# One-core linear attention and two channel mixers: loads spaced out, level masks as a bitwise and, decay products on GpSimd

## The chip, the cores and the metric

The kernel runs on one core of a Trainium2 chip. The metric is device time in microseconds of one execution; the kernel before took 908.53 us (median of three runs, 905.54 to 910.15).

## The reference, cut to what matters

Four batches, eight heads, 768 tokens, head width 48, everything float32. Three stages follow each other:

```
state = alpha[t] * state + outer(k[t], v[t]);  y[t] = q[t] @ state        # linear attention, per head
x = y, heads side by side (384 wide)
xk, xr = token-shifted mixes of x;  k = relu(xk @ w_k);  x = sigmoid(xr @ w_r) * (k*k @ w_v)
u = x + token mixing of x through U, V (rank 32);  out = u + relu(u @ w_ch1) @ w_ch2
```

## The kernel before, in words

**Units.** One unit of attention is half a batch: 384 tokens of 8 heads, n = 2b + half, eight units in all. Q and K lie feature by token in `QK` with two groups g = 0, 1 of 768 columns, and alpha in `T`. The causal attention inside a chunk of 128 tokens is built up over levels of doubling blocks: TensorE multiplies K and Q blocks (`in_half`, L419, 96 small matmuls a level), VectorE copies the wanted blocks of the result into `Pm` under a byte mask (`keep`, L1029), then multiplies Q and K by the decay products (L1060 for level step 0, L1065 for the others) and doubles the decay products themselves (`double_T`, L1035). `keep` has three forms, by the block width B: B = 1 (levels 0 and 1), B = 2 (level 2, with the two inner axes exchanged), B of 4 and more (levels 3 to 5). Levels 6 and 7 are copied by ScalarE (L787, L791). `Pm` starts as zeros (L1243; the second unit has its own `Pm_2`, L1296), so that masked places stay zero. After the levels TensorE turns K (L475), multiplies `Pm` by v (L483), forms the change of state per chunk (L510), VectorE carries the states along (`end_states`, L1082 and L1095), and TensorE adds what comes from the state (L526).

**Weights in two parts.** Every product of the mixers is three fp32r matmuls, high x high, low x high, high x low (L594 to L596). So each weight is split once: ScalarE makes the high part (L928), and a subtraction makes the low part: on VectorE for six of the pieces of w_k and w_v (L1239), on GpSimd for w_r, one piece each of w_k and w_v, and all twelve pieces of w_ch1 and w_ch2 (L1302).

**Order of the work.** Each engine's program is written out by hand. Unit 0 runs alone. After that, attention of the next unit is cut into 13 steps (a generator), and the plans `FIRST`, `BESIDE1`, `BESIDE_T`, `BESIDE2`, `BESIDE3` say how many steps come ahead of each slice f of the mixers, on all engines alike. `channel_mix` is the first mixer (8 slices f, with hidden squares made by VectorE at L1170 and L1173), `mlp` the second (12 slices, L1215). `mix` prepares their inputs (ACT L862, DVE L1148, L1143). Half (0, 0) is straight code, with attention of unit 1 beside it. A hardware loop over b = 0 to 2 then does `channel_mix(b,1)`, `token_mix(b)`, `mlp(b,0)` beside attention of unit (b+1, 0), and `channel_mix(b+1,0)`, `mlp(b,1)` beside unit (b+1, 1). The rest of batch 3 follows with no attention beside it. TensorE meets the steps of `keep`, L1065 and the hidden squares through semaphores; VectorE does them in one queue, in program order.

**The start.** SyncE issues the loads of q, k and alpha of unit 0, then at once all of mu, w_r, w_k, v, V, the six tensors of unit 1, w_v, U and w_ch1 (L339 to L378). w_ch2 is loaded at L355 after unit 1 is done, as its raw copy lies over `Pm_2`. In `attend_first` the first attention step of unit 1 (`next(other)`, its diagonal) stands on TensorE ahead of the turning of K and on VectorE ahead of `end_states` of unit 0. ScalarE makes the high parts of w_v partly after unit 0 (`run(highs)`).

Of the kernel before, what the change touches and what calls it, by code (L numbers as in the profile page):

```python
# [31 lines left out]
U8 = mybir.dt.uint8  # L32
ALU = mybir.AluOpType
# [7 lines left out]
def build(nc, q, k, v, alpha, mu_in, w_k, w_v, w_r, U, V, w_ch1, w_ch2, out):  # L41
# [21 lines left out]
    with ctx:  # L63
# [16 lines left out]
        with ExitStack() as first:  # L80
            def early(name, shape):
                return first.enter_context(nc.sbuf_tensor(name, shape, F32))

            QK_2 = early("QK_2", [P, 2, 2 * S])
            T_2 = early("T_2", [P, 2 * S])
            raw = [early(f"raw_{name}", [P, *shape]) for name, shape in (
                ("k", (KT, F1 * P)), ("r", (KT, DM)), ("v", (F1, DM)), ("1", (KT, F2 * P)))]
            with nc.sbuf_tensor("Pm_2", [P, 2 * NC, 2, P], F32) as Pm_2:
                pass
            raw.append(early("raw_2", [P, F2, DM]))  # L90
            masks = early("masks", [P, 2, MW])
# [11 lines left out]
        level_mask = sb("level_mask", [P, MW], U8)  # L103

# [20 lines left out]
        class Unit:  # L125
            QK: object
            T: object
            Pm: object
# [18 lines left out]
        def states(qk, at):  # L147
# [3 lines left out]
            Unit(QK, T, Pm, [vt[:], by_chunk(x1_flat[:, HC * DM:HC * DM + NC * HP])], [states(QK, 0), states(QK, 1)]),  # L151
            Unit(QK_2, T_2, Pm_2, [vt[:], by_chunk(QK_2[:, 1, 0:NC * HP])], [states(QK_2, 0)] * 2),
            Unit(QK, T, Pm, [vt[:], by_chunk(QK[:, 1, 0:NC * HP])], [states(QK, 0)] * 2),
# [33 lines left out]
        s_zero, s_zero_2 = sem("zero"), sem("zero_2")  # L187
# [4 lines left out]
        s_wld = [sem(f"w{i}_loaded") for i in range(5)]  # L192
# [7 lines left out]
        s_second = pair("second_loaded")  # L200
# [3 lines left out]
        s_qk, s_T = pair("QK_doubled"), sem("T_doubled")  # L204
# [96 lines left out]
        def loaded(eng, n, s, g):  # L301

            if isinstance(n, int) and n == 1:
                eng.wait_ge(s_second[g], 48)
# [11 lines left out]
        def _(sp):  # L316
# [35 lines left out]
            def load_w(i, src, parts):  # L352
                n = src.shape[1]
                for j in range(0, n, n // parts):
                    sp.dma_start(raw[i][:, j:j + n // parts, :], src[:, j:j + n // parts, :]).then_inc(s_wld[i], 16)  # L355
# [12 lines left out]
            load_w(1, w_r, 1)  # L368
            load_w(0, w_k, 3)
            load_v(0, 0, 0)  # L370
            load_v(0, 0, 1)
            sp.dma_start(V_raw, V).then_inc(s_V, 16)
            for g in range(2):
                sp.dma_start(part(units[1].K(), g), k[0, 1, g]).then_inc(s_second[g], 16)
                sp.dma_start(part(units[1].Q(), g), q[0, 1, g]).then_inc(s_second[g], 16)
                sp.dma_start(part(T_2[0:HR], g), alpha[0, 1, g]).then_inc(s_second[g], 16)
            load_w(2, w_v, 2)
            sp.dma_start(u_sb[:], U).then_inc(s_U, 16)  # L378
            load_w(3, w_ch1, 3)
# [34 lines left out]
        def _(pe):  # L414
# [63 lines left out]
            def own(n, g, h, c, z, q0, q1):  # L478

                u = unit(n)  # L480
                for e in range(2):
                    cc, keys = h * HC + c, slice(z * HS, (z + 1) * HS)
                    mm = pe.matmul(y_bank(n, g, h)[e * HS:e * HS + D, c * P + q0:c * P + q1], u.vt[g][keys, cc, e, :],  # L483
                                   u.Pm[keys, g * NC + cc, e, q0 - z * HS:q1 - z * HS],
# [74 lines left out]
            def attend_first(steps, other):  # L559
# [4 lines left out]
                next(other)  # L564
# [25 lines left out]
                from_state(n, half, 1)  # L590

# [125 lines left out]
            def mlp(b, half, step, plan, acc_free, turns=()):  # L717
                s = 2 * b + half
                for f in range(F2):
                    step(plan[f])  # L720
                    if f == 0 and half == 0:
                        pe.wait_ge(s_plo, NR + 2 + 2 * N1)
# [52 lines left out]
        def _(act):  # L775
            def levels(n):
                Pm = unit(n).Pm
# [23 lines left out]
            def attention(b, half):  # L801
# [3 lines left out]
                act.wait_ge(s_T, LV * (n + 1))  # L805
                for g in range(2):
                    for h in range(2):
# [16 lines left out]
            def attend_first(steps, highs):  # L824


                for _ in range(ML + 2):
                    next(steps)
                    next(highs, None)
                next(steps)  # L830
                next(highs)
# [98 lines left out]
            def early_weights():  # L930

                act.wait_ge(s_wld[1], 16)
                for n in range(NR):
                    high(n, *PIECES[n][:2])
                yield
# [3 lines left out]
                yield  # L939
                act.wait_ge(s_wld[0], 48)  # L940
                for n in range(NR, NR + NK):
                    high(n, *PIECES[n][:2])
                    if n % 2 == 0:
                        yield
                yield
                yield
                yield
                act.wait_ge(s_wld[2], 32)
                for n in range(NR + NK, NR + 2 * NK):
                    high(n, *PIECES[n][:2])  # L950
                    if n == NR + NK:
                        yield

            def later_weights():

                act.wait_ge(s_wld[3], 48)
# [4 lines left out]
            def last_weights():  # L961

                act.wait_ge(s_y[1], 4)
                act.wait_ge(s_split, 64 * KT)
                act.wait_ge(s_wld[4], 48)
                for n in range(NE + N1, NE + 2 * N1):
                    high(n, *PIECES[n][:2])
# [3 lines left out]
            highs = early_weights()  # L971
            attend_first(levels(0), highs)
            steps = together(attention(0, 1), later_weights(), [1] * 13, N1)
            step = stepper(steps)
            step(START)
            run(highs)
# [26 lines left out]
        def _(dve):  # L1003
# [399 lines left out]
```

## Time and profile before

| | |
|---|---|
| profiled execution, own time | 905.27 us |
| its span, first to last instruction | 903.5 us |
| TensorE busy | 801.7 us (89%) |
| VectorE busy | 475.6 us (53%) |
| ScalarE / GpSimd busy | 272.5 / 39.4 us |
| mean granted TensorE clock | 0.941 of full |

A busy share says how much of the span an engine had an instruction under way. TensorE is near full over most of the span; the holes lie in the first 176 us and once in each half of the loop.

### The profile page before, as it was taken

To read this page: it belongs to the slowest core of one execution; us is meant where nothing else is said; L and a number is where in the kernel's file an instruction comes from. 1 tells how busy PE (TensorE), PEld (TensorE's weight loads), DVE (VectorE), ACT (ScalarE), POOL (GpSimd) and SP (SyncE) were. 2 spreads that over 40 slices of the span, in tenths; PEclk is the share of its full clock that TensorE was granted. 3 is DMA by queue.
4 is the path that set the end of the run, shared out by engine and by line. 5 is a ranking of instruction groups with operands and counts; after the bars stand their busy time and mean duration, and the time that the engine had idled before them with its cause. 6 is when DMAs were issued, how large, how long until landed. Compare 5 with 4: busy or idle time off the path is not lost.

```text
span 903.5 us, 24726 instructions
## 1 busy us (share of the span) xinstructions
PE 801.7 (89%) x10680; PEld 744.0 (82%) x10680; DVE 475.6 (53%) x797; ACT 272.5 (30%) x555; POOL 39.4 (4%) x40
## 2 busy tenths in 40 slices
PE   4656985798998998798998999889999899998998
PEld 4556875687998898796997989787899889997998
DVE  6668837864277624765247732676328651533132
ACT  1234334234241413223232333213333142421121
POOL 2040028000000000000000000000000000000000
PEclk9977896899999999889999999889999999999999
DMA  9600024000400012000120004000120000000000
GB/s 273 219 21 3 2 90 141 2 2 16 111 28 3 15 52 89 2 2 15 52 89 1 3 18 108 29 2 1 50 77 28 1 15 8 27 1 1 1 27 26
DMA packets 15602, 37.32 MB, mean 41 GB/s; under 512 B 2544, under 2 KB 6512, under 8 KB 15504
## 3 DMA queue, kind: packets, MB, share of 16 engines
q1 hardware_dynamic: 15408, 35.72, 13.2%
q8 instruction: 88, 1.44, 0.7%
q10 hardware_dynamic: 96, 0.07, 0.0%
q14 instruction: 10, 0.08, 0.0%
HBM read 29.89 MB, written 4.72 MB: 38 GB/s over the span
## 4 chain that ended last, share of the span: by engine, by line
PE 76%; DVE 16%; issue 5%; ACT 2%; DMA 1%; DVEq 0%; SPq 0%; ACTq 0%
PE acc L594 11%; PE acc L595 10%; PE acc L596 10%; PE hps L594 9%; PE hps L595 8%; PE hps L596 8%; PE aps L419 7%; DVE Pm L1029 4%; DVE QK L1065 4%; PE aps L483 2%; PE aps L526 2%; PE hps L682 2%; DVE T L1035 1%; PE aps L475 1%; DVE QK L1060 1%
## 5 line engine op out<-in xcount | busy, mean ns | idle before, releaser
L1215 DVE SCALAR_TENSOR_TENSOR hid_l<-hps,hid_h 128x384 fp32r<-128x384 f32 x96 | 53.5, 557 | 215.6 <-ACT hid_h L922 215.6
L1065 DVE TENSOR_TENSOR QK<-QK,T 112x768 f32<-112x768 f32 x96 | 92.2, 974 | 42.2 <-PE aps L419 36.7
L419 PEld LDWEIGHTS aps<-QK 48*64 48x64 f32 x4704 | 82.4, 146 | 37.1 <-issue 37.1
L922 ACT ACTIVATE hid_h<-hps 128x384 fp32r<-128x384 f32 x96 | 47.2, 492 | 207.9 <-PE hps L596 207.9
L419 PE MATMUL aps<-QK 48*64 48x32 f32 x4704 | 88.1, 230 | 23.5 <-DVE Pm L1029 9.9
L594 PE MATMUL hps<-in_h,w_h 128*128 128x384 f32 x288 | 100.2, 348 | 1.0 <-DVE in_l L1191 0.9
L596 PE MATMUL hps<-in_h,w_l 128*128 128x384 f32 x288 | 96.9, 337 | 0.0
L595 PE MATMUL hps<-in_l,w_h 128*128 128x384 f32 x288 | 96.9, 336 | 0.0
L596 PE MATMUL acc<-w_h,hid_l 128*128 128x384 f32 x288 | 96.4, 335 | 0.0
L594 PE MATMUL acc<-w_h,hid_h 128*128 128x384 f32 x288 | 96.3, 334 | 0.0
L595 PE MATMUL acc<-w_l,hid_h 128*128 128x384 f32 x288 | 96.2, 334 | 0.0
L888 ACT ACTIVATE tmp<-hps 128x384 f32<-128x384 f32 x64 | 31.5, 492 | 187.1 <-PE hps L596 156.8
L594 PE MATMUL acc<-wv_h,hid_h 128*128 128x384 f32 x192 | 68.9, 359 | 21.1 <-DVE hid_l L1173 21.1
L1029 DVE COPY_PREDICATED Pm<-level_mask,aps 128x384 f32<-128x384 uint8 x84 | 78.7, 937 | 0.0
L594 PE MATMUL hps<-in_h,wk_h 128*128 128x384 f32 x192 | 72.1, 376 | 3.4 <-DVE in_l L1143 3.4
L595 PE MATMUL acc<-wv_l,hid_h 128*128 128x384 f32 x192 | 67.1, 349 | 0.0
L596 PE MATMUL acc<-wv_h,hid_l 128*128 128x384 f32 x192 | 67.0, 349 | 0.0
L596 PE MATMUL hps<-in_h,wk_l 128*128 128x384 f32 x192 | 66.9, 348 | 0.0
L595 PE MATMUL hps<-in_l,wk_h 128*128 128x384 f32 x192 | 66.9, 348 | 0.0
L594 PEld LDWEIGHTS acc<-wv_h,hid_h 128*128 128x128 f32 x192 | 38.1, 199 | 26.8 <-DVE hid_l L1173 23.6
L1170 DVE TENSOR_TENSOR hid_h<-tmp 128x384 fp32r<-128x384 f32 x64 | 37.0, 578 | 41.8 <-ACT tmp L888 41.8
L594 PEld LDWEIGHTS hps<-in_h,w_h 128*128 128x128 f32 x288 | 54.6, 190 | 4.9 <-issue 2.2
(147 smaller groups left out, 1365.9 us busy)
## 6 DMA issues: line engine op xcount, KB each, us to landing
QK<-in_k SPq DMA_DIRECT2D x16, 336.0 KB, 4.2
QK<-in_q SPq DMA_DIRECT2D x16, 336.0 KB, 5.4
T<-in_alpha SPq DMA_DIRECT2D x16, 336.0 KB, 5.7
raw<-in_w_ch SPq DMA_DIRECT2D x6, 768.0 KB, 13.5
out<-x SPq DMA_DIRECT2D x24, 192.0 KB, 1.9
vt<-in_v SPq DMA_DIRECT2D x8, 288.0 KB, 4.3
QK<-in_v SPq DMA_DIRECT2D x7, 288.0 KB, 2.8
raw_k<-in_w_k SPq DMA_DIRECT2D x3, 512.0 KB, 9.8
```

Of the source, the lines that this page charges most:

```text
L419: return pe.matmul(to[z * HS:(z + 1) * HS, at:at + W2], u.K()[rows, cols], queries(u.Q()[rows, cols]), start=True, stop=True)
L483: mm = pe.matmul(y_bank(n, g, h)[e * HS:e * HS + D, c * P + q0:c * P + q1], u.vt[g][keys, cc, e, :], u.Pm[keys, g * NC + cc, e, q0 - z * H ...
L526: mm = pe.matmul(y_bank(n, g, h)[rows, c * P:(c + 1) * P], before, u.Q()[rows, t0:t0 + P], start=False, stop=(c == HC - 1))
L594: pe.matmul(o, a[0], b[0], start=first, stop=False)
L595: pe.matmul(o, a[0], b[1], start=False, stop=False)
L596: return pe.matmul(o, a[1], b[0], start=False, stop=last)
L888: nc.scalar.activation(tmp[:, 0, :], hps[f % 2][:, 0:HT], ACT.Relu).then_inc(s_rel, 1)
L922: nc.scalar.activation(hid[0][:, f % 2, :], hps[f % 2][:, 0:HT], ACT.Relu).then_inc(s_rel2, 1)
L1029: nc.vector.copy_predicated(to, m, src).then_inc(s_keep, 1)
L1065: nc.vector.tensor_tensor(qk, qk, t, ALU.mult).then_inc(s_qk[g], 1)
L1170: nc.vector.tensor_tensor(hid[0][:, f % 2, :], tmp[:, 0, :], tmp[:, 0, :], ALU.mult).then_inc(s_hh, 1)
L1215: nc.vector.scalar_tensor_tensor(out=hid[1][:, f % 2, :], in0=hps[f % 2][:, 0:HT], scalar=0.0, in1=hid[0][:, f % 2, :].bitcast(F32), op0=A ...
```

## The change

- **Loads**: nearly every load after the first six waits for the landing of the one two before it, so that two are under way; w_ch2 is loaded after w_ch1, not after unit 1. Semaphores are per part.
- **Masks**: `whole_mask` holds 0 or -1 as int32 (two small GpSimd instructions). For levels 0 and 1 `keep` writes all places with `bitwise_and` of the PSUM result and this mask, from PSUM to `Pm`. Levels 2 to 5 keep `copy_predicated`; the exchanged form for B = 2 is gone, so level 2 uses the form of levels 3 to 5. The clearing of `Pm` and all of `Pm_2` are gone; all units share `Pm`.
- **Decay products**: `double_T` leaves VectorE. GpSimd has a stream `attention(n)` for each unit, with the same products per group g (14 instructions a unit), waiting for `s_Ke[g]` or `s_qk[g]`, with a loop of its own over b.
- **Unit 1's diagonal**: `next(other)` moves behind unit 0's `from_state(…,1)` on TensorE and behind `end_states` and the copies of y on VectorE.
- **Low parts**: the twelve pieces of w_ch1 and w_ch2 go from GpSimd to VectorE: six in the steps beside half (0, 0) (`LOWS`), six after it (`last_lows`).
- **High parts**: ScalarE makes w_r, w_k and V ahead of unit 0's level copies and w_v between these and the copies of y; w_ch1 follows `HIGHS`. The high parts of w_ch2 stay after `mix(0,1,0)`.
- **Plan**: `FIRST` brings unit 1's steps forward: [0,1,2,1,2,1,2,1,2,0] becomes [0,1,2,2,2,2,2,1,0,0].

```
-                if B == 1:
-                    to, src = to[:, :, :, 0], src[:, :, :, 0]
-                    m = m.unsqueeze(1).to_broadcast([P, 2 * NC, k])
-                elif B == 2:
-                    to, src = (x.rearrange("p c n b -> p c b n") for x in (to, src))
-                    m = m.unsqueeze(1).unsqueeze(1).to_broadcast([P, 2 * NC, B, k])
-                else:
-                    m = m.unsqueeze(2).unsqueeze(1).to_broadcast([P, 2 * NC, k, B])
+                if lev < 2:
+                    m = whole_mask[:, mask_at(lev):mask_at(lev) + k].unsqueeze(1).to_broadcast([P, 2 * NC, k])
+                    nc.vector.tensor_tensor(to[:, :, :, 0].bitcast(I32), src[:, :, :, 0].bitcast(I32), m,
+                                            ALU.bitwise_and).then_inc(s_keep, 1)
+                    return
+                m = m.unsqueeze(2).unsqueeze(1).to_broadcast([P, 2 * NC, k, B])
                 nc.vector.copy_predicated(to, m, src).then_inc(s_keep, 1)
...
+            def attention(n):                                    # GpSimd
+                t = unit(n).T[0:HR]
+                for l in range(LV):
+                    B = 1 << l
+                    for g in range(2):
+                        part_t = part(t, g)
+                        t_left, t_right = part_t[:, B - 1:S:2 * B], part_t[:, 2 * B - 1:S:2 * B]
+                        if l == 0:
+                            pool.wait_ge(s_Ke[g], n + 1)
+                        else:
+                            pool.wait_ge(s_qk[g], LV * n + l + 1)
+                        to = t_right
+                        if l == LV - 1:
+                            to = T_end[:, g * NC:(g + 1) * NC]
+                            ge(pool, s_st[g], 4 * n)
+                        nc.gpsimd.tensor_tensor(to, t_right, t_left, ALU.mult).then_inc(s_T[g], 1)
+                    yield
...
-            load_w(1, w_r, 1)
-            load_w(0, w_k, 3)
+            sp.wait_ge(s_ldq[1], 16)
+            load_part(rw, w_r, 0, KT, s_wr)
+            sp.wait_ge(s_lda[1], 16)
+            load_part(kw, w_k, 0, 1, s_wk[0])
+            sp.wait_ge(s_wr, 16)
+            load_part(kw, w_k, 1, 1, s_wk[1])
...
             sp.wait_ge(s_y[0], 2)
             load_v(0, 1, 0)
+            for i in range(3):
+                sp.wait_ge(s_w1[i], 16)
+                load_part(w2w, w_ch2, i * F2 // 3, F2 // 3, s_w2[i])
             load_v(0, 1, 1)
             move_split(0, 1)
-            sp.wait_ge(s_y[1], 4)
-            load_w(4, w_ch2, 3)
...
             run(steps)                                           # VectorE, after channel_mix(0, 0)
+            last_lows()
```

## Rows read from the trace of the kernel before

**Rows 1.** Windows by part of the program: start:end, length, busy us, clock, DMA

```profile
0.00:66.00 66.00, 38.62 (x1028) 35.08 (x1028) 41.93 (x61) 15.52 (x27) 15.69 (x28) 0.91 0.57 176
66.00:133.00 67.00, 55.64 (x993) 51.48 (x994) 43.93 (x72) 29.26 (x58) 2.79 (x2) 0.83 0.06 16
133.00:176.00 43.00, 25.99 (x367) 23.83 (x366) 36.14 (x37) 14.45 (x27) 20.90 (x11) 0.76 0.31 100
176.00:783.00 607.00, 567.83 (x7665) 525.16 (x7665) 318.36 (x563) 186.89 (x391) 0.00 (x0) 0.96 0.11 31
```

**Rows 2.** TensorE in order of time; in brackets the idle before, and its releaser

```profile
279.98 0.69 PE L594 MATMUL acc<-wv_h,hid_h 128*128 128x384 f32 x1 [3.06 <-DVE hid_l L1173]
...
359.98 1.32 PE L419 MATMUL aps<-QK 48*64 48x32 f32 x75 [2.21 <-issue]
...
374.29 1.68 PE L419 MATMUL aps<-QK 48*64 48x32 f32 x96 [0.39 <-DVE Pm L1029]
383.91 0.44 PE L594 MATMUL acc<-wv_h,hid_h 128*128 128x384 f32 x1 [3.06 <-DVE hid_l L1173]
```

**Rows 3.** Windows around two of these waits

```profile
276.00:286.00 10.00, 6.94 (x119) 6.23 (x118) 6.05 (x9) 1.01 (x2) 0.00 (x0) 0.83 0.00 0
380.00:394.00 14.00, 10.94 (x156) 9.87 (x157) 9.18 (x14) 2.04 (x4) 0.00 (x0) 0.76 0.01 1
```

**Rows 4.** VectorE in order of time, ahead of the wait at 276.9

```profile
264.47 1.01 DVE L1029 COPY_PREDICATED Pm<-level_mask,aps 128x384 f32<-128x384 uint8 x1
...
276.36 1.84 DVE L1029 COPY_PREDICATED Pm<-level_mask,aps 128x384 f32<-128x384 uint8 x1
277.81 1.07 DVE L1035 TENSOR_TENSOR T<-T 112x384 f32<-112x384 f32 x1
...
285.76 0.57 DVE L1029 COPY_PREDICATED Pm<-level_mask,aps 128x384 f32<-128x384 uint8 x1
```

**Rows 5.** Groups of instructions: busy, mean ns, idle before

```profile
L1035 DVE TENSOR_TENSOR T<-T 112x768 f32<-112x768 f32 x8 | 8.7, 1092 | 0.0
L1184 DVE TENSOR_TENSOR x<-acc,x 128x384 f32<-128x384 f32 x24 | 12.3, 553 | 9.4 <-PE acc L596 9.4
```

**Rows 6.** One line on VectorE: duration in ns, least, median, most

```profile
L1045 DVE TENSOR_TENSOR QK<-QK,T x16: 553/558/2205, 7.5 to 685.4; 112x384 f32<-112x384 f32 x16
```

**Rows 7.** The chain that ended last, 22 to 66 us: start, length, what

```profile
22.75 2.94 issue
...
30.04 2.56 issue
...
37.29 1.56 issue
...
65.04 2.29 ACT wv_h L928 x3
```

**Rows 8.** GpSimd and VectorE beside each other, 48 to 57 us

```profile
51.79 2.12 POOL L1302 TENSOR_TENSOR wv_l<-raw_v,wv_h 128x768 fp32r<-128x768 f32 x1
...
52.16 1.01 DVE L1029 COPY_PREDICATED Pm<-level_mask,aps 128x384 f32<-128x384 uint8 x1
52.98 1.75 DVE L1035 TENSOR_TENSOR T<-T 112x768 f32<-112x768 f32 x1
```

**Rows 9.** TensorE and VectorE in order of time, 56 to 163 us

```profile
56.89 1.09 PE L526 MATMUL hps<-QK 48*48 48x128 f32 x8 [4.21 <-DVE carry L1095]
...
132.40 1.87 DVE L1170 TENSOR_TENSOR hid_h<-tmp 128x384 fp32r<-128x384 f32 x1 [4.10 <-ACT tmp L888]
...
153.10 4.28 DVE L1045 TENSOR_TENSOR QK<-QK,T 112x384 f32<-112x384 f32 x2
...
144.75 1.51 PE L419 MATMUL aps<-QK 48*64 48x32 f32 x48 [5.10 <-DMA QK<-in_k]
...
162.89 0.69 PE L594 MATMUL hps<-in_h,wk_h 128*128 128x384 f32 x1 [2.84 <-DVE in_l L1143]
```

**Rows 10.** DMA issues: kind, count, KB each, us to landing

```profile
QK<-in_k SPq DMA_DIRECT2D x16, 336.0 KB, 4.2
```

More of the change, by code:

```diff
@@ L32 @@
 U8 = mybir.dt.uint8
+I32 = mybir.dt.int32
 ALU = mybir.AluOpType
@@ L199, in build @@
         s_ldq, s_ldk, s_lda, s_ldv = (pair(f"{n}_loaded") for n in "qkav")
[L200 removed]
+        s_q2, s_k2, s_a2 = (pair(f"second_{n}_loaded") for n in "qka")
         s_dg, s_Ke = pair("even_diagonal"), pair("K_even_ready")
@@ L350, in move_split, with load_part @@
                                      unit(n).y_split()[e * HS + 16 * i:e * HS + 16 * (i + 1), :]).then_inc(s_split, 16)
[L352 to L355, printed above, removed]
+            def load_part(raw_w, src, i, n, done):
+                sp.dma_start(raw_w[:, i:i + n, :], src[:, i:i + n, :]).then_inc(done, 16)
             def store(b, half):
@@ L367, in _ @@
             sp.dma_start(mu[:, 0:2, :], mu_in).then_inc(s_mu, 16)
-            load_w(1, w_r, 1)
-            load_w(0, w_k, 3)
+            sp.wait_ge(s_ldq[1], 16)
[4 more added lines that the diff above has]
+            load_part(kw, w_k, 1, 1, s_wk[1])
+            sp.wait_ge(s_wk[0], 16)
+            load_part(kw, w_k, 2, 1, s_wk[2])
+            sp.dma_start(V_raw, V).then_inc(s_V, 16)
+            sp.wait_ge(s_wk[1], 16)
             load_v(0, 0, 0)
+            sp.wait_ge(s_wk[2], 16)
             load_v(0, 0, 1)
[L372 to L377, printed above, removed]
-            sp.dma_start(u_sb[:], U).then_inc(s_U, 16)
-            load_w(3, w_ch1, 3)
+            sp.wait_ge(s_ldv[0], 16)
+            load_part(vw, w_v, 0, F1 // 2, s_wv[0])
+            sp.wait_ge(s_ldv[1], 16)
+            load_part(vw, w_v, F1 // 2, F1 // 2, s_wv[1])
+            Q2, K2 = units[1].Q(), units[1].K()
+            sp.wait_ge(s_wv[0], 16)
+            sp.dma_start(part(K2, 0), k[0, 1, 0]).then_inc(s_k2[0], 16)
+            sp.wait_ge(s_wv[1], 16)
+            sp.dma_start(part(Q2, 0), q[0, 1, 0]).then_inc(s_q2[0], 16)
+            sp.wait_ge(s_k2[0], 16)
+            sp.dma_start(part(K2, 1), k[0, 1, 1]).then_inc(s_k2[1], 16)
+            sp.wait_ge(s_q2[0], 16)
+            sp.dma_start(part(Q2, 1), q[0, 1, 1]).then_inc(s_q2[1], 16)
+            sp.wait_ge(s_k2[1], 16)
+            sp.dma_start(part(T_2[0:HR], 0), alpha[0, 1, 0]).then_inc(s_a2[0], 16)
+            sp.wait_ge(s_q2[1], 16)
+            sp.dma_start(part(T_2[0:HR], 1), alpha[0, 1, 1]).then_inc(s_a2[1], 16)
+            sp.dma_start(u_sb[:], U).then_inc(s_U, 16)
+            sp.wait_ge(s_a2[0], 16)
+            load_part(w1w, w_ch1, 0, 1, s_w1[0])
+            sp.wait_ge(s_a2[1], 16)
+            load_part(w1w, w_ch1, 1, 1, s_w1[1])
+            sp.wait_ge(s_w1[0], 16)
+            load_part(w1w, w_ch1, 2, 1, s_w1[2])
             move_split(0, 0)
@@ L590, in attend_first @@
                 from_state(n, half, 1)
+                next(other)
             def three(o, a, b, first, last):
@@ L822, in attention, with attend_first @@
                     yield
[L824 to L831, printed above, removed]
+            def attend_first(steps):
+                first_weights()
+                run(steps)
+                next_weights()
                 for g in range(2):
@@ L1045, in levels @@
                     nc.vector.tensor_tensor(k_even, k_even, t_odd, ALU.mult).then_inc(s_Ke[g], 1)
-                keep(n, 0, 0)
-                dve.wait_ge(s_Ke[1], n + 1)
-                double_T(n, 0)
-                keep(n, 0, 1)
+                for e in range(2):
+                    keep(n, 0, e)
                 yield
@@ L1122, in attend_first @@
                         ).then_inc(s_kt[g], 1)
-                dve.wait_ge(s_zero_2, 1)
-                next(other)
                 end_states(0, 0, 0)
@@ L1132, in attend_first @@
                         nc.vector.tensor_copy(to, y_bank(0, g, h)[rows, 0:HT]).then_inc(s_xe, 1)
+                next(other)
             def mix(b, half, what, between=lambda: None):
@@ L1302, in low @@
                 nc.gpsimd.tensor_tensor(w_lo, src, w_hi.bitcast(F32), ALU.subtract).then_inc(s_plo, 1)
-            pool.wait_ge(s_qk[1], LV)
+            run(attention(0))
             for n in (*range(NR + 1), NR + NK):
@@ L1312, in _ @@
             pool.wait_ge(s_vst, 3)
-            pool.wait_ge(s_y[1], 4)
-            for n in range(NE, NE + 2 * N1):
-                low(n, n)
-FIRST = [0, 1, 2, 1, 2, 1, 2, 1, 2, 0]
+            run(attention(1))
+            with pool.Fori(1, NB) as b:
+                run(attention(2 * b))
+                run(attention(2 * b + 1))
+FIRST = [0, 1, 2, 2, 2, 2, 2, 1, 0, 0]
 BESIDE1 = [1, 1, 1, 0, 1, 1, 0, 1, 1, 0]
```

121 lines of the change are left out of this document (55 added, 66 removed).

## The prediction

> **What bounds the kernel now.** I read the windows by part of the program first, since a mean over the span hides where time is lost. From 176 to 783 us TensorE is busy 567.8 of 607 us at clock 0.96, [rows 1]; the 120.5 us after it have no attention and are not touched. Ahead of that it is idle 27.4, 11.4 and 17.0 us in three parts that end at 176 us, at clocks of 0.91, 0.83 and 0.76. So there are two places: the opening, and whatever opens the 39 us of holes in the loop. TensorE's own order of time shows these: one wait of 3.06 us in each half with attention beside it, always for the hidden square's low part on VectorE [rows 2]; it occurs five times after 176 us, at 280, 384, 492, 596 and 703. Behind each the granted clock falls to 1.2 GHz for a while: the stretch reads 0.83 over 10 us in three cases, 0.76 over 14 us in two [rows 3], which is 1.7 and 3.4 us of work lost each, 11.9 in all. VectorE's rows show why it is late: from 262 (or 372) on it runs with no gap, and hid_h and hid_l stand in its queue behind two level-2 keeps of 1.8 us and a T of 1.07 us [rows 4]. VectorE at 53% busy is thus the bound for some 18 us of every half.
>
> **Masks.** A keep of level 0 or 1 takes 1.01 us and one of level 2 1.84, one of level 3 0.57, for the same 384 elements [rows 4]; starts of neighbours are 0.92, 1.78 and 0.47 us apart, as neighbours overlap by about 0.1. The bitwise and is a two-operand instruction with 384 elements. The nearest rows are the PSUM add, 0.553 us [rows 5], and the product with a step of two elements, 0.558 us [rows 6]: 0.47 net. Upper bound: no gain, 0.92. I take 0.47, since both output step and source are as in these rows. Saved: 0.45 each, four a unit. Level 2 in the plain form writes pairs of elements; the level-0 form writes every second element, also two in each four, so I put it at 0.93, with bounds 0.47 (level 3) and 1.78 (no gain). Saved: 0.85 each, two a unit.
> The Trainium skill, "SBUF — State Buffer", section on port mapping, says two hits in a 16-byte line suffice for full bandwidth; by that rule level 2 would cost 0.47 too. The level-0 keep has two hits in a line and takes twice a level-3 keep, so for this instruction the row speaks against the rule; by the rule about 0.4 us more would be saved a keep, most of it where no wait is left.
>
> **T on GpSimd.** VectorE loses T: 0.99 at step 0 (eight in 8.7 us, one of them stretched to 1.75 [rows 5, 8]), 1.07 at step 1 [rows 4], then 0.5, 0.33, 0.24, 0.2, 0.18. On GpSimd a two-operand subtraction of 768 columns takes 2.12 us [rows 8], 2.75 ns a column; T of one group has 384, 192, 96, ... products, so 1.06, 0.53, 0.26 us and little after: 4.1 us a unit. Bounds: as on VectorE below, three times as much above, since no row has GpSimd with a step. It is needed one step later, over 3 us on, so it hides. What it touches is VectorE: while GpSimd ran its 2.12 us, VectorE's T, with two SBUF inputs, took 1.75 in place of 1.0, whereas the keep beside it, with PSUM as source, took its usual 1.01 [rows 8]. So only products and in_l/hid operations can be held up, for at most one GpSimd instruction. By the queue order T(0,g) runs beside the two ands and touches in_l by up to 1 us, T(1,g) and later ones run beside the keep that follows their product: nothing. I take 0.3 us a unit.
> The Trainium skill, "SBUF — State Buffer", section on who interferes with whom, says that a DVE instruction with two SBUF inputs and a GpSimd one that reads SBUF exclude each other fully. The rows above agree for the two-input case, and with the exemption of one-input ones. Taken as a rule against this change, all GpSimd time could land on VectorE; that is the first rival.
>
> **The loop, five halves.** In the three halves of the 280 kind VectorE's full run starts before step 0 (262), and loses 0.9 + 0.99 + 0.9 + 1.7 + 1.07 = 5.5 us ahead of hid_l, more than the 3.06 wait. In the two of the 384 kind the run starts at 372, and loses 0.9 + 1.7 + 1.07 = 3.7, against 3.06 plus 0.39 that TensorE itself comes earlier, its wait for the level-1 keep being gone [rows 2]; after handoffs I leave 0.3. Sum: 3 x 3.06 + 2 x 3.15 = 15.5. Of the 11.9 lost by the clock I take 9, as other gaps (2.21 us, instruction supply, at the loop's end [rows 2], and one before u is turned) stay. Small ones: 0.5. Together 25. If an edit brings less than its share, the wait comes back with the clock.
>
> **Opening, unit 0 (to 47).** VectorE's run up to 22 us loses 0.9 + 0.8 + 0.9 + 1.7, of which TensorE's two matmul halves of 1.5 us a step leave 3. Behind it stand three gaps of TensorE in which nothing but instruction supply is late, 2.94 + 2.56 + 1.56 = 7.1 [rows 7], while the loads fill the DMA engines (they end with them). Spaced loads bring between nothing and all of it, or lose if loads come late: 16 landings up to the first part of w_ch1, two under way, 4.2 us each [rows 10], end at about 10 + 16 x 2.1 = 44 us, ahead of the move of y behind it in SP's queue (58 before, about 50 after); w_r, w_k, w_v land by 30 and are wanted at 40 or later. With a third more each it would be 55, and the move about 5 us late. I take 1.5, so 4.5 for this part.
> **47 to 68.** The diagonal's work on VectorE (48.78 to 55.4, stretched by GpSimd [rows 8]) leaves the path from K's turning to the states. What is late next is TensorE: turning the states of group 1 ends at 52.7, so its 4.21 us gap before the state product [rows 9] goes and some of the 1.2 GHz time after it: 6. High parts of w_v and one of w_ch1 behind the last y, 2.29 [rows 7] + 0.82, go: 3.1. Given back: products and ands of the diagonal ahead of mix, 4 x 0.47 = 1.9. Together 7.
> **68 to 139.5.** The run of VectorE from 78.3 to 102.8 loses 0.9 + 1.7 + 2.3 (T of steps 1 to 4) = 4.9. The plan that brings steps forward changes only order: VectorE has 27 us of work to the end of step 6, TensorE 18 us. At 133 TensorE waits 3.0 us for hid_l while GpSimd's subtractions stretch hid_h to 1.87 [rows 9] and runs at 1.2 GHz for 3 us: 4.5 back, as no subtraction is left there. Six w_ch1 subtractions at 0.87 move to VectorE where it is 60 to 70% idle: 1 lost (0 to 5). Together 8.4.
> **139.5 to 162.89.** This is 23.4 us for TensorE, with a 5.1 us wait for K behind w_ch2 and two-input operations of 2 us each on VectorE [rows 9]. After, K is there, and the chain is VectorE's: mix 2.6, three products 1.5, six w_ch2 subtractions 5.2, two sums of mix 1.1, products and ands 1.9, in_l 0.5, ACT and sum 1.2, in_l twice 1.1, handoffs 0.2: 15.3. Saved 8.1. The wait of 2.5 at 173 goes as in the loop: 2.5. Without that chain's subtractions it would be 13; beside GpSimd nothing now.
>
> **Sum.** 4.5 + 7 + 8.4 + 8.1 + 2.5 + 25 = 55.5. Own time 905.3 - 55.5 = 849.8; the median of the runs is 3.3 above the profiled one, so 853.
>
> **Rivals.**
> 1. *The port takes it back.* GpSimd's T of steps 0 and 1 is 3.2 us a unit; if each holds up a two-input operation in VectorE's full run, eight units lose 25 us: about 879. For: rows 8 and 9. Against: the queue order puts keeps, which aren't held up, beside nearly all of them.
> 2. *The masks cost as before.* If the and takes 0.92 and level 2 1.78, only T leaves the run: the loop's waits shrink by 3 x 2.06 + 2 x 1.07 = 8.3 and the clock gives 4, so 12.3 in place of 25; the opening loses about 3.5: 869. For: no row has an int32 operation or the pair form. Against: same element counts as in rows 5.
> 3. *Slower.* GpSimd's product with a step costs three times the contiguous one, 8 ns an element: T is 12.3 us a unit, T(0,g) 3.1 each. They then stand before the step-0 products and hold up mix: the run grows by 9.3 - 5.5 = 3.8 in each of 6 halves, with the clock 23 to 30 on top of the present time, and about 10 in units 0 and 1, against 28 kept in the opening: about 915. It turns at some 8 ns an element. For: the step is new. Against: the row shows 2.75.
> 4. *The start stays as it is.* If instruction supply and late loads bind TensorE up to the first mix as before, 4.5 + 7 go: 865. For: the gaps end with the loads. Against: the 4.21 us gap waits for VectorE, not for a load [rows 9].
>
> **Chances.** Forecast 0.64, first 0.13, second 0.10, fourth 0.07, slower 0.04; 0.02 for no change. Between 0.5% either way this kernel can't be told from itself. Range: rivals 1, 2 and 4 reach to 879; below, all supply gaps, the whole clock and no port loss are 5.6 + 2.9 + 2.4 + 3 = 14, so to 839; rounding errors of the hand count widen it: 834 to 882. The forecast's own range is 838 to 865. Faster 0.93, same 0.02, slower 0.05.
>
> **What would show it.** On TensorE's order of time no wait over 0.5 us for L1173 in the loop; clock near 1 where it read 0.83; level-2 keeps near 0.93 and ands near 0.56; T on GpSimd near 1.06 and 0.53, and no L1143 or L1065 above 1.2 us beside it; mix of half (0,0) begins by 57; f = 0 of half (0,1) about 30 us earlier, near 133. Wrong: hid_l waits that stay with the old length, in which case the run of VectorE was not what I took it for, or TensorE waiting for SP's move of y.

## The result and the profile after

The changed kernel takes 854.24 us (median; 851.68 to 855.22), against 909.29 of the kernel before: ratio 0.940, 95% interval [0.936, 0.943]. The forecast of 853 with "faster" was right. The profiled execution took 855.14 us with a span of 853.4, and between the two profiled executions the gain is 50.1 us where the prediction added up 55.5: the opening gave 24.4 us instead of 30.5, the loop 26 instead of 25. That the median still came within 1.3 us of the forecast is luck, see below.

One line of TensorE separates the two well: the 24 matmuls with `v_stack` in the low-rank product of the MLP, the first behind the opening, the last near the end. Before and after (count; least, median and longest duration in ns; first and last start in us):

```profile
L700 PE MATMUL acc<-hid_h,v_stack x24: 334/414/689, 207.0 to 822.3; 96*128 96x384 f32 x24
```

```profile
L723 PE MATMUL acc<-hid_h,v_stack x24: 334/416/686, 182.6 to 771.9; 96*128 96x384 f32 x24
```

Below, the first number is called the opening (207.0 to 182.6) and the difference the loop (615.3 to 589.3). In the ten kernels below that leave the loop as the change made it, it is 589.1 to 590.0, so it repeats from profile to profile within 1 us. The opening does not: unit 0's y is ready at 43 us in e5, e7 and e8 and at 47 after the change, though the code up to there is the same.

Windows by part of the program, as in [rows 1] (start:end, length, busy us of TensorE, its weight loads, VectorE, ScalarE and GpSimd, then clock, DMA share and GB/s):

```profile
0.00:58.00 58.00, 37.25 (x1031) 33.86 (x1031) 31.67 (x57) 18.78 (x33) 21.18 (x45) 0.95 0.77 240
58.00:121.00 63.00, 54.98 (x991) 50.44 (x991) 42.80 (x69) 25.86 (x52) 6.44 (x12) 0.88 0.17 47
121.00:149.00 28.00, 21.23 (x348) 19.97 (x349) 23.16 (x38) 13.55 (x25) 2.95 (x4) 0.76 0.01 3
149.00:733.00 584.00, 561.30 (x7686) 519.51 (x7685) 291.11 (x526) 188.66 (x395) 41.05 (x80) 0.98 0.12 33
```

In the loop TensorE is busy 96% at clock 0.98, where it was 94% at 0.96. The three parts of the opening are shorter, and still at 0.95, 0.88 and 0.76.

TensorE's order of time, where [rows 2] had 3.06 us, and the window around the wait, for [rows 3]:

```profile
252.08 0.44 PE L617 MATMUL acc<-wv_h,hid_h 128*128 128x384 f32 x1 [0.31 <-DVE hid_l L1172]
...
351.69 0.44 PE L617 MATMUL acc<-wv_h,hid_h 128*128 128x384 f32 x1 [0.30 <-DVE hid_l L1172]
```

```profile
248.00:258.00 10.00, 9.69 (x142) 9.08 (x141) 7.36 (x12) 2.65 (x6) 1.62 (x3) 1.00 0.00 0
348.00:358.00 10.00, 9.70 (x142) 9.09 (x141) 7.37 (x11) 3.06 (x6) 1.87 (x4) 1.00 0.01 2
```

VectorE and GpSimd in order of time ahead of that wait, for [rows 4]:

```profile
237.98 1.02 DVE L1038 TENSOR_TENSOR Pm<-aps,whole_mask 128x384 int32<-128x384 int32 x2
238.91 1.04 DVE L1142 TENSOR_TENSOR in_l<-tmp,in_h 128x384 fp32r<-128x384 f32 x1
...
243.55 0.96 DVE L1064 TENSOR_TENSOR QK<-QK,T 112x768 f32<-112x768 f32 x1 [1.16 <-PE aps L442]
...
247.35 0.95 DVE L1069 TENSOR_TENSOR QK<-QK,T 112x768 f32<-112x768 f32 x1
248.22 1.03 DVE L1042 COPY_PREDICATED Pm<-level_mask,aps 128x384 f32<-128x384 uint8 x1
```

```profile
237.68 1.86 POOL L1325 TENSOR_TENSOR T<-T 112x384 f32<-112x384 f32 x2 [53.10 <-DVE QK L1052]
248.39 0.54 POOL L1325 TENSOR_TENSOR T<-T 112x192 f32<-112x192 f32 x1 [8.85 <-DVE QK L1069]
```

An and takes 0.55 us, a level-2 keep 1.03; T on GpSimd takes 0.93 (step 0) and 0.54 (step 1) a group. In these rows only in_l, the low part of a mixer's input, is stretched by GpSimd beside it, to 1.04. And VectorE is not continuously busy any more: at 243.55 it waited 1.16 us for TensorE.

The opening. TensorE in order of time, all idle times over 0.8 us between 20 and 140 us (in brackets, with what ended them), then the chain around the first mix (start, length, what) and what SyncE waited for between 40 and 60 us (total, times, longest):

```profile
25.67 0.32 PE L442 MATMUL hps<-QK 48*64 48x32 f32 x3 [1.10 <-issue]
32.29 0.21 PE L442 MATMUL acc<-QK 48*64 48x32 f32 x1 [2.12 <-issue]
56.46 0.69 PE L617 MATMUL acc<-wr_h,in_h 128*128 128x384 f32 x1 [6.21 <-DVE in_l L1142]
72.17 2.35 PE L442 MATMUL aps<-QK 48*64 48x32 f32 x96 [2.59 <-DVE Pm L1042]
82.94 1.81 PE L442 MATMUL aps<-QK 48*64 48x32 f32 x96 [0.90 <-DVE Pm L1042]
90.95 1.24 PE L449 MATMUL aps<-QK 48*64 48x64 f32 x48 [1.32 <-ACT Pm L809]
106.02 0.86 PE L506 MATMUL aps<-Pm,QK 64*48 64x128 f32 x24 [1.49 <-issue]
127.75 0.68 PE L617 MATMUL acc<-wr_h,in_h 128*128 128x384 f32 x1 [3.16 <-DVE x L1183]
135.34 1.60 PE L442 MATMUL aps<-QK 48*64 48x32 f32 x96 [1.24 <-DVE Pm L1038]
139.10 0.69 PE L617 MATMUL hps<-in_h,wk_h 128*128 128x384 f32 x1 [2.16 <-DVE in_l L1142]
```

```profile
45.93 0.56 DVE T L1130
46.49 0.49 DVE xT L1130
46.98 0.50 SPq L348
47.52 0.83 SPq L348
48.39 5.54 DMA xT<-T
54.01 0.62 ACT tmp L882
54.65 0.63 DVE tmp L1147
```

```profile
SPq L352 <- DMA raw<-in_w_ch: 6.8, 2, 4.4
```

The 7.1 us of supply gaps of [rows 7] (idle times of TensorE that end with "issue") are 3.2; the wait for K at 144.75 and the two-input operations of 2 us of [rows 9] are gone; f = 0 of half (0, 1), the first slice of its mixer, starts at 139.10 instead of 162.89. The row with 6.21 has a forerunner of 5.80 us before the change:

```profile
69.69 0.69 PE L594 MATMUL acc<-wr_h,in_h 128*128 128x384 f32 x1 [5.80 <-DVE in_l L1143]
```

What stands ahead of it is new: the chain of the changed kernel runs through the move of y (pieces of 24 KB), whose transfer takes 5.54 us.

### The profile page after: what moved, and what is told of

It reads as the page before. It is cut to its first block, busy times and chain, and to the rows that moved or that the text cites. A ratio compares the mean times of both kernels' runs of the same rounds, so it can differ in the third digit from the quotient of the medians.

```text
span 853.4 us, 24863 instructions
## 1 busy us (share of the span) xinstructions
PE 788.8 (92%) x10680; PEld 732.5 (86%) x10680; DVE 423.9 (50%) x752; ACT 272.7 (32%) x555; POOL 71.6 (8%) x141
## 4 chain that ended last, share of the span: by engine, by line
PE 80%; DVE 10%; issue 5%; ACT 2%; DMA 2%; SPq 0%; DVEq 0%; ACTq 0%
PE acc L617 11%; PE acc L619 11%; PE acc L618 11%; PE hps L617 10%; PE hps L618 9%; PE hps L619 9%; PE aps L442 7%; PE aps L506 3%; PE aps L549 2%; DVE QK L1069 2%; PE hps L705 2%; DVE Pm L1042 1%; PE aps L533 1%; PE acc L442 1%; DVE hid_h L1169 1%
## 5 line engine op out<-in xcount | busy, mean ns | idle before, releaser
L1325 POOL TENSOR_TENSOR T<-T 112x384 f32<-112x384 f32 (+5 forms) x96 | 51.8, 543 | 560.2 <-DVE QK L1052 310.0
L442 PEld LDWEIGHTS aps<-QK 48*64 48x64 f32 x4704 | 77.0, 138 | 24.5 <-issue 24.3
L442 PE MATMUL aps<-QK 48*64 48x32 f32 x4704 | 82.8, 223 | 12.1 <-issue 7.4
L617 PE MATMUL acc<-wv_h,hid_h 128*128 128x384 f32 x192 | 66.1, 344 | 2.5 <-DVE hid_l L1172 2.4
L619 PE MATMUL acc<-wv_h,hid_l 128*128 128x384 f32 x192 | 64.6, 337 | 0.0
L618 PE MATMUL acc<-wv_l,hid_h 128*128 128x384 f32 x192 | 64.5, 336 | 0.0
L618 PEld LDWEIGHTS hps<-in_l,w_h 128*128 128x128 f32 x288 | 54.7, 190 | 0.0
```

What stands on the lines that cost most here:

```text
L442: return pe.matmul(to[z * HS:(z + 1) * HS, at:at + W2], u.K()[rows, cols], queries(u.Q()[rows, cols]), start=True, stop=True)
L617: pe.matmul(o, a[0], b[0], start=first, stop=False)
L618: pe.matmul(o, a[0], b[1], start=False, stop=False)
L619: return pe.matmul(o, a[1], b[0], start=False, stop=last)
L1325: nc.gpsimd.tensor_tensor(to, t_right, t_left, ALU.mult).then_inc(s_T[g], 1)
```

## The experiments

The opening and loop of each are from the same line of TensorE in one profile; times are medians, and the ratio is to the kernel before as timed beside it (medians of 905.8 to 910.5). Since unit 0's y is ready anywhere between 43 and 47 us without any edit there, a difference of a few us between two openings is not by itself a gain; the intervals and the lengths of single stretches say more.

| kernel | time, us | ratio, 95% | opening | loop |
|---|---|---|---|---|
| before | 909.3 | 1 | 207.0 | 615.3 |
| after | 854.24 | 0.940 [0.936, 0.943] | 182.6 | 589.3 |
| e1 masks only | 878.13 | 0.970 [0.966, 0.974] | 200.4 | 594.3 |
| e2 T on VectorE | 859.54 | 0.952 [0.946, 0.959] | 178.6 | 597.1 |
| e3 level 2 as before | 872.19 | 0.962 [0.958, 0.966] | 183.9 | 603.6 |
| e4 loads at once | 858.87 | 0.949 [0.945, 0.953] | 182.2 | 589.8 |
| e5 old plan | 850.28 | 0.936 [0.932, 0.940] | 178.5 | 589.6 |
| e6 quiet move | 851.60 | 0.936 [0.931, 0.941] | 184.4 | 589.7 |
| e7 w_ch2 lows on GpSimd | 858.82 | 0.946 [0.941, 0.951] | 185.0 | 589.8 |
| e8 early w_ch2 | 849.93 | 0.935 [0.930, 0.939] | 177.3 | 589.1 |
| e10 move first | 851.82 | 0.934 [0.928, 0.941] | 179.1 | 590.0 |
| e11 e10 and e8 | 847.57 | 0.932 [0.927, 0.936] | 175.9 | 589.3 |
| e12 e11 and e5 | 844.96 | 0.930 [0.926, 0.934] | 170.5 | 589.6 |
| e13 e12, first T on VectorE | 847.30 | 0.936 [0.932, 0.939] | 170.7 | 589.7 |

**e1, masks only** (the kernel before, with this part of the diff alone):

```
+                if lev < 2:
+                    m = whole_mask[:, ...]
+                    nc.vector.tensor_tensor(to[:, :, :, 0].bitcast(I32), ..., m, ALU.bitwise_and)
+                    return
...
-                elif B == 2:
-                    to, src = (x.rearrange("p c n b -> p c b n") for x in (to, src))
...
```

> The kernel before with one part of the change: bitwise and for levels 0 and 1, level 2 in the plain form. T stays on VectorE. Queue theory (VectorE's full run ahead of hid_l sets the 3.06 us waits, whatever shortens it counts): 3.5 us leave the run in the halves of the 280 kind, so their waits vanish, 2.6 leave it in the 384 kind, so about 0.8 stays; 14.4 us and some 9 of the clock in the loop, 5 to 7 in the opening: about 880. Rival (the waits go only once T has left VectorE as well): under 10 us gained, about 900.

Measured 878.13. TensorE's waits in the two kinds of half:

```profile
271.99 0.44 PE L596 MATMUL acc<-wv_h,hid_h 128*128 128x384 f32 x1 [0.99 <-DVE hid_l L1173]
371.27 0.44 PE L596 MATMUL acc<-wv_h,hid_h 128*128 128x384 f32 x1 [0.96 <-DVE hid_l L1173]
```

The masks alone bring 21 of the loop's 26 us and 6.6 of the opening. The wait fell by 2.1 us in both kinds of half, where the expectation had none left in the 280 kind and 0.8 in the other.

**e2, T on VectorE** (the changed kernel, T doubled by `double_T` as before, one instruction for both groups).

> The changed kernel with T back on VectorE, one instruction for both groups as before, nothing else. Queue theory: the 280 kind has 2.4 us of slack and T puts back 2.06, so no wait there; the 384 kind waits about 1.3 in place of 0.3; 2 us in the loop, 4 in the opening, where VectorE's run is longer: about 860. Rival (T's busy time on VectorE counts in full, 8 x 3.4): about 881. Port rival (GpSimd's T costs VectorE as much as it frees): 854 or less.

Measured 859.54. The waits are 1.35 and 0.98:

```profile
250.49 0.44 PE L617 MATMUL acc<-wv_h,hid_h 128*128 128x384 f32 x1 [1.35 <-DVE hid_l L1184]
351.38 0.44 PE L617 MATMUL acc<-wv_h,hid_h 128*128 128x384 f32 x1 [0.98 <-DVE hid_l L1184]
```

So the 280 kind does not have the slack that was expected. T on GpSimd is worth 7.8 us in the loop, net of what GpSimd costs VectorE there (0.5 us on in_l in the 280 kind). Of these 4.5 are the five waits; no lower clock follows them (1.00 in each 4 us behind all five), so the other 3.3 lie elsewhere. The opening is 4 us shorter without it in this profile (see e13).

**e3, level 2 as before** (the changed kernel with the exchanged form of B == 2 back).

> The changed kernel with the exchanged form of level 2 (B = 2) back, nothing else. Queue theory: 1.7 us come back to VectorE's run in each half; the 280 kind has slack for most of it, the 384 kind waits 2.0 in place of 0.3, with part of the clock's loss; 3 in the opening: 860 to 866. Rival (this edit is neutral, the and does it all): 854 to 856.

Measured 872.19, outside what was expected. The keep is 1.86 us again, and both kinds of half wait 2.03:

```profile
257.44 0.49 PE L617 MATMUL acc<-wv_h,hid_h 128*128 128x384 f32 x1 [2.03 <-DVE hid_l L1176]
...
360.39 0.44 PE L617 MATMUL acc<-wv_h,hid_h 128*128 128x384 f32 x1 [2.03 <-DVE hid_l L1176]
```

```profile
254.00:264.00 10.00, 7.97 (x124) 7.17 (x123) 5.87 (x9) 1.02 (x2) 0.98 (x2) 0.83 0.00 0
357.00:367.00 10.00, 7.97 (x131) 7.12 (x129) 7.38 (x11) 2.04 (x4) 1.63 (x3) 1.00 0.01 2
```

The loop is 14.3 us longer. Five waits longer by 1.72 us are 8.6 of it. The other 5.7 are not simply "the clock behind the wait": it fell behind the first of the five (0.83 above) and stayed at 1.00 behind the other four. Lower clock is found elsewhere: over 12 us around TensorE's first three waits of 2.4 us for x, behind token mixing, it reads 0.57, 0.72 and 0.72 here against 0.86 three times after the change, where these waits are as long. Why it stays low longer there is open. The expected slack in the 280 kind did not exist here either.

**e4, loads at once** (the changed kernel, SyncE's waits between the loads ahead of the move left out).

> The changed kernel with the waits between the opening's loads taken out, so that they are all issued at once as before; w_ch2 stays where the change put it. Supply theory: TensorE's gaps for instruction supply, 7.1 us in three, 1.1 us in the changed kernel, come back, so unit 0's levels end 5 to 6 us later; against it the move of y no longer stands behind w_ch1, 3.6 us earlier: together 856 to 857. Rival (spacing has nothing to do with supply): the gaps stay away and only the move gains: 851.

Measured 858.87, above both expectations; opening 182.2. The supply gaps are back, 1.75 + 1.74 + 3.66 + 1.85 = 9.0, and unit 0's last product ends at 42.8 instead of 37.55. But the wait for in_l is 3.69 instead of 6.21, and the first r matmul (the mixer's product with w_r, where the next stage of TensorE starts) comes at 56.85 against 56.46. So in this pair of profiles spacing brings 5 us in unit 0, and the next stage does not get it. Over the runs it does: the median is 4.6 us above the changed kernel and the intervals lie apart. The profiled run, at 855.03, was the fastest of the four.

**e5, old plan** (`FIRST = [0, 1, 2, 1, 2, 1, 2, 1, 2, 0]` in the changed kernel).

> The changed kernel with the old order of unit 1's steps beside half (0,0)'s units (one step more in units 4, 6 and 8, none in the last). Theory (steps set too close together): with the new plan TensorE waits 2.59, 0.90, 1.32 and 0.61 us in 68 to 95 on a level's P of the unit being doubled, since DVE's and ScalarE's steps of two levels outlast one r and s matmul of the mixers; with the old plan these waits shrink by about 3 to 4 us, the end of half (0,0) comes at about 119 to 120 instead of 122.8, but the last steps then reach into the cover that the first r matmul of (0,1) needs, so that f=0 of half (0,1) comes within 1 us of 139.1: span 850 to 853, time 852 to 856. Rival (new plan is what brought the opening its gain): f=0 of half (0,1) comes 4 us or more later, at 143 or more, time 858 to 861.

Measured 850.28, 4 us under the changed kernel: its four times (849.2 to 851.66) lie just below the other's four (851.68 to 855.22), though the intervals of the ratios still overlap. From the first r matmul to the sums behind half (0, 0) (122.2, after the change 126.0) is 3.4 us shorter; f = 0 of (0, 1) starts at 135.2, 3.9 us earlier, where I had expected it within 1 us of 139.1. Of the waits, not those of 2.59 and 0.90 went (2.71 and 0.90 are there), but the 1.32, 0.48 and 1.49 behind 90 us. So the time came out below the theory's range, and the gain came by other waits than I named. By the trace, the new plan cost 3.4 us in this stretch.

**e6, quiet move** (w_ch1's third part and w_ch2 issued when the move of y has landed).

> The changed kernel with the third part of w_ch1 and all of w_ch2 issued only after the move of y of units 0 and 1 has landed. Theory (the small move stands in the 16 queues behind bulk loads that were issued 0.7 us before it): its transfer takes about 2 us instead of 5.54, the first sum of the mixer stage comes at about 51 instead of 54.65, the first r matmul at about 53 instead of 56.46, f=0 of half (0,1) at 136 to 137 instead of 139.1, time 850.5 to 852.5. Rival (what is late there is not the move but the steps of ScalarE and DVE beside it): the transfer shortens and first r matmul moves by less than 1 us, time 853.5 to 855. A second rival: w_ch1's third part now lands after unit 2 of half (0,0) wants it, a wait of TensorE of 2 us or more between 62 and 70, time 854 to 857.

Measured 851.60 (846.7 to 857.2), and the transfer did not shorten: 5.1 us a move, with two parts of w_ch1 ahead of it. The theory and its first rival both had it shorten. Together with e10 this shows that what was issued ahead counts, not what is issued behind. The first r matmul came 2.1 us earlier, and the profiled opening was still 1.8 longer, at a clock of 0.81 from 58 to 121 us; with times 10 us apart, nothing clear follows for the gain.

**e7, w_ch2's low parts on GpSimd** (the changed kernel, the six subtractions behind unit 1's T on GpSimd, `last_lows` gone from VectorE).

> The changed kernel with the low parts of w_ch2 subtracted on GpSimd again, behind unit 1's T. Theory (the term 139.5 to 162.89 of the prediction: six subtractions of about 0.88 us on DVE, 5.3 us, in place of six of 1.8 to 2.1 us on GpSimd, which ScalarE's last conversions pace): the second half's mixers start with the lows still under way, f=0 of half (0,1) at 142 to 146 instead of 139.1, time 857 to 861. Rival (GpSimd's six run beside DVE's last steps of unit 1 at once, nothing waits for them): f=0 at 137 or earlier, time 850 to 853.

Measured 858.82. GpSimd, and VectorE beside it:

```profile
124.83 11.68 POOL L1331 TENSOR_TENSOR w_l<-raw,w_h 128x768 fp32r<-128x768 f32 x6 [32.34 <-ACT w_h L949]
```

```profile
128.98 3.79 DVE L1148 SCALAR_TENSOR_TENSOR tmp<-xT,mu,tmp 128x384 f32<-128x384 f32 x2 [2.97 <-ACT tmp L883]
132.70 4.23 DVE L1053 TENSOR_TENSOR QK<-QK,T 112x384 f32<-112x384 f32 x2
136.85 1.01 DVE L1039 TENSOR_TENSOR Pm<-aps,whole_mask 128x384 int32<-128x384 int32 x2
```

Two sums of mix take 3.79 instead of 1.14, two products 4.23 instead of 1.02, while the two ands behind them, which have PSUM as source and T on GpSimd beside them, take their usual 1.01. From the first w_ch2 conversion to f = 0 is 17.4 us instead of 13.7. The Trainium skill, "SBUF — State Buffer", section on who interferes with whom, lets two-input VectorE instructions and GpSimd exclude each other; this trace agrees.

**e8, early w_ch2** (two of the six high and low pieces in the unit before the last of half (0, 0)):

```
+EARLY = [0, 0, 0, 0, 0, 0, 0, 0, 2, 0]
...
-            channel_mix(0, 0, step, FIRST)                       # ScalarE; VectorE alike, with last_lows()
+            last = last_weights()
+            channel_mix(0, 0, also(step, last, EARLY), FIRST)
...
```

> The changed kernel with the first two of w_ch2's six high and low pieces converted while half (0,0)'s unit before the last runs, instead of behind all steps. Theory (between 121 and 139 ScalarE's conversions and DVE's subtractions are the chain): two pieces less in it, f=0 of half (0,1) 1.7 to 2 us earlier at about 137.3, time 852 to 853. Rival (another chain ends there, so the pieces only lengthen the steps that they stand in front of): f=0 at 139 to 140, time 854 to 856.

Measured 849.93, below the expectation; its four times are all below the changed kernel's four, the intervals overlap. The same stretch is 11.9 us instead of 13.7, f = 0 starts at 135.9, and the clock over the 28 us from 121 reads 0.88 instead of 0.76. The six pieces were in the chain. Of the 3.2 us by which f = 0 is earlier, 1.5 come ahead of the conversions, from what is open; from f = 0 to the line with `v_stack` is 41.4 us instead of 43.5, at clock 0.96 instead of 0.90.

**e10, move first** (the changed kernel):

```
             load_part(w1w, w_ch1, 0, 1, s_w1[0])
-            sp.wait_ge(s_a2[1], 16)
-            load_part(w1w, w_ch1, 1, 1, s_w1[1])
-            sp.wait_ge(s_w1[0], 16)
-            load_part(w1w, w_ch1, 2, 1, s_w1[2])
             move_split(0, 0)
             sp.wait_ge(s_y[0], 2)
             load_v(0, 1, 0)
+            sp.wait_ge(s_split, 32 * KT)
+            load_part(w1w, w_ch1, 1, 1, s_w1[1])
+            load_part(w1w, w_ch1, 2, 1, s_w1[2])
```

> The changed kernel with SyncE's move of y of unit 0 issued ahead of w_ch1's second part, and w_ch1's second and third part issued once it has landed. Theory (the spaced loads put SyncE's wait for w_ch1's first part, landed at 46 to 47, ahead of the move in its order; where unit 0's y is ready at 43 to 44, as in three of the five profiles, the move still starts at 47 and ends at 53 to 54): the move is issued as soon as y is ready and has one bulk load ahead of it instead of three, it lands at 47 to 50, the first sum of the mixer stage comes 3 to 5 us earlier than the 54.65 of the changed kernel, f=0 of half (0,1) at 134.5 to 137 instead of 139.1; time 849 to 852 (the changed kernel 854.2). Rival (loads of w_ch1 and w_ch2, 3 us later, are then late): TensorE or ScalarE waits for raw between 60 and 80 for 2 us or more, time 853 to 857.

Measured 851.82 (843.1 to 854.8, not apart from the changed kernel's times). The issues of the move, after and here (KB each, us to landing):

```profile
xT<-T SPq DMA_DIRECT2D x3, 24.0 KB, 4.8
```

```profile
xT<-T SPq DMA_DIRECT2D x3, 24.0 KB, 2.7
```

The first sum of VectorE for the mixer comes at 51.2 instead of 54.65 (52.9 to 54.65 in the profiles of after, e5, e7 and e8, which leave this part alone), the opening ends at 179.1 instead of 182.6, and no wait for w_ch1 appears. In the profiles of e5 and e8 y was ready by 43 and still moved at 47, behind SyncE's wait for w_ch1's first part: their faster unit 0 was lost there. In the changed kernel's own profile y was ready at 46.97, just behind that landing (46.8), so there only the longer transfer counts.

**e11 and e12, combined.**

> Move of y first (as before) and two pieces of w_ch2 converted beside the unit before the last of half (0,0). Theory (the two gains lie in different stretches, 47 to 57 and 121 to 139, and add up: about 3 and about 2 to 4 us): time 846 to 849. Rival (ScalarE and DVE become the bound of 58 to 121 and take the second back): 849 to 852.

> The same and the old order of unit 1's steps. Theory (the waits of TensorE of 0.90, 1.32 and 0.61 us on levels set two to a unit go, and the conversions ahead of f=0 still have their cover): 843 to 847, 1 to 4 us under the kernel without the old order. Rival (the steps moved back and the two pieces now meet in the same unit of half (0,0), so TensorE waits there): within 1 us of the kernel without it, or above it.

Measured 847.57 and 844.96. By medians the gains of e10 and e8 add in full (2.4 + 4.3 us, measured 6.7), and e5's 4.0 brings 2.6 more; by the ratios each of the three edits alone still overlaps with the change, and e12 does not. The openings of 175.9 and 170.5 are partly chance, as y was ready at 47.9 in the one profile and at 42.5 in the other. e12 is the fastest kernel here, 7.0% under the one before; its interval [0.926, 0.934] ends below that of the change, [0.936, 0.943]. Its profile over the stretch in which the second half's mixers start:

```profile
121.00:149.00 28.00, 26.94 (x485) 25.39 (x486) 23.61 (x38) 8.96 (x18) 4.41 (x7) 0.92 0.01 2
```

**e13, T of units 0 and 1 on VectorE** (e12 besides).

> The kernel with the move first, the two early pieces and the old order of unit 1's steps, and besides T of the first two units doubled on VectorE (one instruction for both groups), the loop's on GpSimd. Theory (in units 0 and 1 GpSimd's small products stand in the chain of a level or beside a mix of VectorE, which a shared port stretches to 1.04 us; with T on VectorE throughout, the first r matmul of the mixers came 2.1 us and f=0 of half (0,1) 3.1 us earlier than in the changed kernel, although that profile's move still stood behind the loads): 842 to 844.5, 0.5 to 3 us under the kernel without it (845.0). Rival (the gain seen then was a difference in when the loads landed, and with it gone VectorE is the later engine in the opening): 845 to 847.

Measured 847.30, in the rival's range, with the profiled openings 170.7 here and 170.5 in e12: no gain. That e2's shorter opening was chance in the end of unit 0 fits this, but is not shown.

## Why the prediction was right

The direction and the size came out, and so did the loop, by nearly the mechanism laid out. The agreement of 853 with 854.24 is closer than the working deserves. The sum of 55.5 gave an own time of 849.8, and the profiled execution took 855.14. The prediction added 3.3 us because the median of the runs before lay that far above the profiled one; after the change the median lies 0.9 below it. So a sum 5.4 us too high met an offset that did not hold. By its own terms, from the two traces:

| part | predicted | measured |
|---|---|---|
| unit 0 | 4.5 | 9.1 (last product's end 46.68 to 37.55) |
| 47 to 68 | 7 | 4.1 (first sum 67.88 to 54.65) |
| 68 to 139.5 | 8.4 | 3.4 (last matmul of half (0, 0) ends at 139.64 and 123.06) |
| 139.5 to 162.89 | 8.1 | 7.2 |
| wait at 173 | 2.5 | 0.6 |
| loop | 25 | 26 |
| sum | 55.5 | 50.4 |

- **Masks and T, prices.** Ands 0.55 (0.56 meant), level 2 1.03 (0.93), T on GpSimd 0.93 and 0.54 (1.06 and 0.53), in_l beside it 1.04: near what was set. The later steps of T cost more than set, 7.4 us a unit in all instead of 4.1, where nothing waits. One reading behind the prices was wrong: the keeps' neighbours start 0.81 (levels 0 and 1) and 1.45 to 1.50 us apart (level 2), not 0.92 and 1.78, so an and frees 0.34 and not 0.45, and level 2 its 0.85 only with the next product and hid_h, which also get shorter. The rivals of masks at their old price and of GpSimd at 8 ns an element fall with these rows; that of the port fell with the waits of 0.31, and e2; that of an opening bound as before falls with the 13.2 us of its first two parts. (The chances of the four faster cases add up to 0.94, not 0.93.)
- **Loop.** The sum held, one step of its working did not: "In the three halves of the 280 kind VectorE's full run starts before step 0 (262), and loses ... 5.5 us". Already before the change that run has a gap, which [rows 4] leave out:

```profile
266.56 0.62 DVE L1148 SCALAR_TENSOR_TENSOR tmp<-xT,mu,tmp 128x384 f32<-128x384 f32 x1 [0.69 <-ACT tmp L862]
```

  The run that counts starts with the first step-0 product in both kinds, behind TensorE's level-1 matmuls: after the change VectorE waits there (1.16 at 243.55), so the level-0 ands and T(0) ahead of it only make slack. It is thus 11 us long before the change in every half, not "some 18". From that product to hid_l is 11.05 us before, 8.60 in e1, 9.64 in e3 and 7.92 after, alike in both kinds: 3.1 us less, of which the two level-1 ands are 0.7, level 2's form 1.7 (e3) and T of step 1 0.7. The wait falls by 0.4 less than that, since TensorE itself comes earlier by its 0.39 of [rows 2]: 3.06 to 0.98 in e1, to 0.31 after. The rule laid out for the 384 kind thus held for all five halves. e3 shows level 2's form to be the largest edit taken back alone, 14.3 of 26 us; the ands alone were not tested. As for the sizes: the five waits gave 13.8 us (15.5 predicted). An estimate for the clock, the missing share times the length over the loop in stretches of 4 us, is 24.0 us before and 13.4 after, so 10.6 (9 predicted).
- **Unit 0.** "I take 1.5" of 7.1 us of supply gaps was too low: 3.8 went in this profile, and 9.0 are there without the spacing (e4). The other 5.3 of the 9.1, by subtraction, are VectorE's run, where I had 3.
- **47 to 68.** The step that failed: "16 landings ... end at about 44 us, ahead of the move of y behind it in SP's queue". The first part of w_ch1 landed at 45 to 47, and the move had two more parts ahead of it in the DMA queues: 5.54 us, not the 1.9 of before. The text named this wait as what would prove it wrong and put 5 us on it if every landing took a third longer; a slower transfer of the move had no term. e10 moves it ahead: 2.7 us a move, and the first sum 1.7 to 3.5 us earlier.
- **68 to 139.5.** "The plan that brings steps forward changes only order" failed: two steps to a unit make TensorE wait for VectorE and ScalarE. e5 gets 3.4 us back there, which is most of the missing 5.0.
- **139.5 to 162.89.** The chain was the one laid out, six subtractions of 0.88 us included (5.29 in the trace); e7 and e8 move it both ways, by +3.7 and -1.8.
- **Wait at 173.** It is gone, but only 0.6 us came of it: the 10 us around f = 0 run at 0.51, against 0.75 before (161.8 to 171.8):

```profile
138.00:148.00 10.00, 8.90 (x115) 8.40 (x116) 7.45 (x13) 2.63 (x6) 0.54 (x1) 0.51 0.01 2
```

The saving was counted without the clock of its own stretch. Ahead of f = 0 TensorE had been idle for 3.16, 1.24 and 2.16 us. Where the chain ahead is shorter the clock comes back: around f = 0 it reads 0.83 in e8 and 1.00 in e12, and from f = 0 to `v_stack` takes 41.4 and 39.9 us instead of 43.5. So part of what e8 and e12 gain is this term.

## What to carry over

A wait that recurs in a loop is worth its length and, at times, lower clock behind it (five of five waits of 3 us here, one of five of 2 us), and only the work between the engine's last own wait and the late result counts toward it; find that start before adding up what an edit saves. Spacing bulk loads shortened the supply gaps here (3.2 us instead of 9.0 in e4), but each wait put into the queue also stands ahead of the small transfers behind it: issue the small one first. A plan that brings steps forward is not neutral; price it by which engine takes two of them at once.

## What was not expected of the hardware

- A small transfer's time follows what was issued ahead of it: 24 KB in 1.9 to 2.2 us before, with no weight load under way; 2.3 to 3.3 with one 768 KB load ahead (e10, e12, e13); 4.1 to 5.7 with two (after, e2, e5 to e8), also without the loads that the change issues behind it (5.1 in e6).
- A predicated copy of the same 384 elements takes 1.86 us where it writes every fourth element, 1.01 where it writes every second, 1.03 in pairs and 0.57 in fours. The Trainium skill, "SBUF — State Buffer", section "Door 1: The DMA port swizzle", says that two hits in a 16-byte line reach full bandwidth. The pairs' 1.03 speaks against it for this instruction.
- The clock behind one wait of TensorE: 1.00 behind all ten of 0.96 to 1.35 us (e1, e2), below 1.00 behind one of five of 2.01 to 2.03 (e3), and behind all five of 3.03 to 3.06 (before).
